# Feed-forward of a routed transformer block: w_out two pieces behind w_in, and two more banks for the first w_in pieces of a group

## What is computed

```python
# attention: q, k, v (4, 12, 448, 64)
attn = sigmoid(q @ k.T / 8 - log(448));  x = attn @ v        # -> (1792, 768)
# experts: each takes 224 tokens, the best logits first
logits = x @ w_gate                                          # (1792, 8)
for idx in argsort(-logits.flatten()):
    tok, e = idx // 8, idx % 8
    if assigned[tok] < 0 and counts[e] < 224: assigned[tok] = e; counts[e] += 1
for e in range(8):
    mask = assigned == e
    y[mask] = relu(x[mask] @ w1[e]) @ w2[e]                  # 768 -> 1024 -> 768
# feed-forward
h = y @ w_in                                                 # 768 -> 2048
g = max(h, 0) + alpha * min(h, 0)
out = g @ w_out                                              # 2048 -> 768
```

## Time and profile before

| | us |
|---|---|
| median of 3 runs (1068.49 to 1069.94) | 1068.9 |
| the profiled execution | 1074.37 |
| its span in the profile | 1072.7 |
| feed-forward of group 0, from its first product to its last | 133.5 |
| of group 1 | 124.7 |
| of group 2 | 124.5 |
| of group 3 | 118.3 |

### The profile page before, as it was taken

How to read it: one execution, slowest core, us unless ns; L and a number is a source line. 1 busy time by engine, 2 the same in 40 slices (tenths; PEclk the granted TensorE clock), 3 DMA queues, 4 the chain that set the end, 5 groups by cost and what they waited for, 6 DMA issues and landing times.

```text
span 1072.7 us, 16546 instructions
## 1 busy us (share of the span) xinstructions
PE 978.1 (91%) x6340; PEld 841.6 (78%) x6340; DVE 588.4 (55%) x1454; ACT 393.0 (37%) x628; POOL 185.5 (17%) x202
## 2 busy tenths in 40 slices
PE   5999999806969999799999999999999999999994
PEld 3555555406969898699989998998899999989993
DVE  2344444597765836966954586497539637211110
ACT  4676777401042123346312224542222355122212
POOL 0010110105150010233301014350100325100001
PEclk9999999956979999999999999999999999999997
DMA  9799997317379586847777855679685446966501
GB/s 213 204 260 270 275 264 228 135 35 236 103 206 363 191 221 181 285 128 223 265 280 235 239 177 130 190 222 368 208 241 195 151 129 188 375 231 220 177 1 51
DMA packets 121476, 222.32 MB, mean 207 GB/s; under 512 B 51424, under 2 KB 69216, under 8 KB 121408
## 3 DMA queue, kind: packets, MB, share of 16 engines
q1 hardware_dynamic: 88064, 120.34, 35.7%
q0 software_dynamic: 21280, 91.59, 27.4%
q10 hardware_dynamic: 12064, 9.47, 3.4%
HBM read 184.84 MB, written 36.52 MB: 206 GB/s over the span
## 4 chain that ended last, share of the span: by engine, by line
PE 83%; DVE 10%; ACT 2%; DMA 1%; issue 1%; POOL 0%; SPq 0%; ACTq 0%; DVEq 0%; POOLq 0%
PE psum L886 19%; PE psum L874 19%; PE psum L821 11%; PE psum L851 11%; PE psum L633 7%; PE psum L617 7%; DVE hits L1348 4%; PE psum L816 2%; PE psum L601 2%; PE psum L846 2%; PE psum L644 1%; DVE unit L1243 1%; DMA stage<-x_rows,tok_idx 1%; PE psum L768 1%; PE psum L652 1%
## 5 line engine op out<-in xcount | busy, mean ns | idle before, releaser
L886 PE MATMUL psum<-g_high,unit 128*128 128x448 f32 x768 | 231.7, 369 | 6.4 <-DVE g_low L1271 6.2
L874 PE MATMUL psum<-y_high,unit 128*128 128x448 f32 x768 | 231.5, 369 | 4.6 <-ACT below L1021 4.3
L886 PEld LDWEIGHTS psum<-g_high,unit 128*128 128x128 f32 x768 | 144.3, 188 | 21.8 <-DVE g_low L1271 9.9
L874 PEld LDWEIGHTS psum<-y_high,unit 128*128 128x128 f32 x768 | 144.3, 188 | 18.8 <-ACT below L1021 5.8
L874 PE MATMUL psum<-y_low,unit 128*128 128x448 f32 x384 | 140.5, 366 | 0.0
L886 PE MATMUL psum<-g_low,unit 128*128 128x448 f32 x384 | 140.5, 366 | 0.0
L1243 DVE TENSOR_TENSOR unit<-raw,unit 128x768 fp32r<-128x768 f32 (+1 forms) x106 | 109.3, 1060 | 39.7 <-ACT unit L994 39.2
L1020 ACT ACTIVATE above<-psum 128x448 f32<-128x448 f32 x64 | 35.0, 546 | 246.2 <-PE psum L874 246.2
L821 PE MATMUL psum<-x_high,unit 128*128 128x224 f32 x672 | 119.8, 280 | 2.9 <-DVE unit L1243 2.9
L1266 DVE SCALAR_TENSOR_TENSOR below<-below,neg_alpha,above 128x448 f32<-128x448 f32 x64 | 43.8, 684 | 138.1 <-ACT below L1021 137.7
L851 PE MATMUL psum<-h_high,unit 128*128 128x224 f32 x672 | 117.2, 278 | 2.5 <-issue 2.5
(11 more groups left out here) (159 smaller groups left out, 1278.7 us busy)
## 6 DMA issues: line engine op xcount, KB each, us to landing
unit<-ffn_parts SPq DMA_DIRECT2D x120, 768.0 KB, 6.4
ffn_parts<-pre_parts POOLq DMA_DIRECT2D x24, 768.0 KB, 5.7
ffn_parts<-unit SPq DMA_DIRECT2D x8, 768.0 KB, 5.5
q_in<-in_q_dram SPq DMA_DIRECT2D x24, 224.0 KB, 3.9
k_in<-in_k_dram SPq DMA_DIRECT2D x24, 224.0 KB, 5.9
v_in<-in_v_dram SPq DMA_DIRECT2D x24, 224.0 KB, 6.2
x_rows<-x_tok POOLq DMA_DIRECT2D x8, 672.0 KB, 5.5
rank_in<-suit_flat POOLq DMA_DIRECT2D x6, 896.0 KB, 14.2
```

Of the source, the lines that this page charges most:

```text
L874: last = pe.matmul(psum[:, IN_BANK, 0:PAIR], w, y[:, c, :], start=(c == 0 and i == 0), stop=(c == DC - 1 and i == 2))
L886: last = pe.matmul(psum[:, OUT_BANK + d, 0:PAIR], w, g[:, m % 2, :], start=(m == 0 and i == 0), stop=(m == FC - 1 and i == 2))
```

## The change

PE's order in a group becomes in 0, in 1, in 2, out 0, in 3, out 1, and so on to in 15, out 13, out 14, out 15. Piece 1 of w_in goes to bank 6 and piece 2 to bank 5, which belong to the result of w_out. So PE waits for `in_taken` only from piece 3 on (which waits that piece 2 is read), and ahead of the last two of the six result banks in out 0. On ACT, `take_in` of piece m now waits that g of piece m - 2 is split, and `round_g` of piece m waits that out m - 2 is done, since with the new order neither follows from what PE has done.

```diff
         def in_unit(q, m):
-            return STEPS * q + 2 * OWN + max(2 * m - 1, 0)
+            return STEPS * q + 2 * OWN + max(2 * m - 2, m)
         def out_unit(q, m):
-            return STEPS * q + 2 * OWN + min(2 * m + 2, 2 * FC - 1)
+            return STEPS * q + 2 * OWN + min(2 * m + 3, FC + m)
+        def in_bank(m):
+            return (IN_BANK, OUT_BANK + DC - 1, OUT_BANK + DC - 2)[m] if m < 3 else IN_BANK
...
             def ffn_in(q, m):
-                if m > 0:
+                if m > 2:
                     pe.wait_ge(in_taken, FC * q + m)
...
             def ffn_out(q, m):
                 for d in range(DC):
+                    if m == 0 and d == DC - 2:
+                        pe.wait_ge(in_taken, FC * q + 3)
...
                 for m in range(FC):
                     ffn_in(q, m)
-                    if m > 0:
-                        ffn_out(q, m - 1)
+                    if m > 1:
+                        ffn_out(q, m - 2)
+                ffn_out(q, FC - 2)
                 ffn_out(q, FC - 1)
...
             def take_in(q, m):
                 act.wait_ge(unit_used, in_unit(q, m) + 1)
+                if m > 1:
+                    act.wait_ge(g_split, FC * q + m - 1)
...
             def round_g(q, m):
                 act.wait_ge(g_made, FC * q + m + 1)
+                if m > 1:
+                    act.wait_ge(unit_used, out_unit(q, m - 2) + 1)
```

More of the change, by code:

```diff
@@ L363, in in_unit @@
         def in_unit(q, m):
-            return STEPS * q + 2 * OWN + max(2 * m - 1, 0)
+            return STEPS * q + 2 * OWN + max(2 * m - 2, m)
         def out_unit(q, m):
-            return STEPS * q + 2 * OWN + min(2 * m + 2, 2 * FC - 1)
+            return STEPS * q + 2 * OWN + min(2 * m + 3, FC + m)
+        def in_bank(m):
+            return (IN_BANK, OUT_BANK + DC - 1, OUT_BANK + DC - 2)[m] if m < 3 else IN_BANK
         def ffn_piece(u):
             k = u % STEPS - 2 * OWN
-            return 0 if k == 0 else 2 * FC - 1 if k == 2 * FC - 1 else 2 * ((k + 1) // 2) if k % 2 == 1 else k - 1
+            if k < 2:
+                return 2 * k
+            if k >= 2 * FC - 2:
+                return 2 * (k - FC) + 1
+            return k + 2 if k % 2 == 0 else k - 2
         def width(u):
@@ L873, in ffn_in @@
                     for i, (w, y) in enumerate(((w_high, y_high), (w_high, y_low), (w_low, y_high))):
-                        last = pe.matmul(psum[:, IN_BANK, 0:PAIR], w, y[:, c, :],
+                        last = pe.matmul(psum[:, in_bank(m), 0:PAIR], w, y[:, c, :],
                                          start=(c == 0 and i == 0), stop=(c == DC - 1 and i == 2))
@@ L1019, in take_in @@
                 act.wait_ge(unit_used, in_unit(q, m) + 1)
-                act.activation(above[:, m % 2, :], psum[:, IN_BANK, 0:PAIR], ACT.Relu)
-                act.activation(below[:, m % 2, :], psum[:, IN_BANK, 0:PAIR], ACT.Relu, scale=-1.0).then_inc(in_taken, 1)
+                if m > 1:
+                    act.wait_ge(g_split, FC * q + m - 1)
+                act.activation(above[:, m % 2, :], psum[:, in_bank(m), 0:PAIR], ACT.Relu)
+                act.activation(below[:, m % 2, :], psum[:, in_bank(m), 0:PAIR], ACT.Relu, scale=-1.0).then_inc(in_taken, 1)
             def round_g(q, m):
                 act.wait_ge(g_made, FC * q + m + 1)
+                if m > 1:
+                    act.wait_ge(unit_used, out_unit(q, m - 2) + 1)
                 act.copy(g_high[:, m % 2, :], below[:, m % 2, :]).then_inc(g_rounded, 1)
```

## The result

The changed kernel takes **1076.1 us** (median of 20 executions, 1070.7 to 1082.0) against 1071.1 (20 executions, 1068.2 to 1073.8) for the kernel before on the same chip: a ratio of **1.0055, 95% interval 1.0041 to 1.007**. It is slower, clear of noise: the medians are 5.0 us apart, and the ratio stands for 5.9 (4.4 to 7.5). The forecast was 0.27% faster, and slower had a chance of 0.05.

The account below looks back on a forecast made before the run. PE, 83% of the span, was taken as the bound through its waits and routing work. Group 3 -1.3, groups 1 and 2 0 each, group 0 -2.5, clock +0.9 make -2.9: 1066.0 us, range 1063.8 to 1068.2.

Parts of the forecast that it names:

- Group 3, -1.3: Feed-forward without routing: the 1.05 us wait before in 1 and one slow start of 0.26 go, gaining 1.3 us.
- Groups 1 and 2, 0 each: Per group, 2.9 us of waits and slow starts saved, 2.9 spent on new waits for flags; bounds -0.6 and +0.6.
- The new waits: PE waits for the flags in groups 1 and 2, since DVE's fill is late: 1.8 us, then 0.7.
- The 0.2 for what a wait costs beyond itself: At each new flags wait, some 0.2 us more, since the two small products run alone after a wait.
- waits of 1.7 never moved it: Argument that the clock stays full in group 0, giving 1065.1 us (1064.3 to 1065.9); chance 0.25.
- Group 0, -2.5: First feed-forward, its end set by DVE: 1.9 us earlier flags plus out 15's 0.4 + 0.26; bounds 0 and 3.4.
- The first pass for expert 3: DVE's pass in group 0 starts 1.1 us earlier on top of the threshold's 0.8, together 1.9.
- The wait at the second threshold: In group 0, PE arrives at 444.7 and thr_rows at 448.3: idle about 3.7 us, up to 4.4.
- The clock in group 0, +0.9: Half clock after PE's wait at the second threshold, partly covered by the flags wait, costs 0.9 us; bounds 0 and 2.9.
- I cost SP's and POOL's queues at nothing: Loads on both queues keep their rule and sizes and only trade places pairwise, so no cost was entered.
- The cover of eleven units: A piece is asked for eleven units ahead, some 40 us at 3.65 each, so loads should not make PE wait.
- The rival "slower": Group 0's PE stays at half clock some 20 us from the second threshold: +4.1, 1073 us; chance 0.05.

Follow-up runs that it names:

- e4: The changed kernel with DVE's weight splits of unit STEPS + 4 held until x has been gathered: 1071.2 us, ratio 0.9996 to the kernel before.
- e8: Changed kernel, w2 gathers first in group 0, fill one unit earlier in groups 1 and 2, idle filler products before group 0's threshold products: 1063.3 us, 0.9928.
- e3: The changed kernel with POOL's w2 gathers issued ahead of storing and spreading the logits, in group 0 only: 1068.9 us, ratio 0.9975.
- e0: The changed kernel once more, unedited, for a second profile: 1076.0 us, ratio 1.0048 to the kernel before.
- e9: e3 with fill one unit earlier in groups 1 and 2, plus e4's hold of DVE: 1060.6 us, ratio 0.9898 to the kernel before.

## Why the prediction was wrong

**Group 3, -1.3: right.** Measured -1.3 in the stretch, -1.4 to the end.

**Groups 1 and 2, 0 each: right in the sum and in the waits, and one cost missing.** The new waits were forecast at 1.8 and 0.7 and came at 1.68 and 0.70, then 1.75 and 0.71; ACT's order was read rightly. The 0.2 for what a wait costs beyond itself is what e4 shows. The pieces of 3.72 us, which the prediction counted as waits and routing work, stand on both sides alike. What was left out is the clock. The row of full clock through waits of 1.7 in the earlier trace rows was taken as a rule ("waits of 1.7 never moved it"). Four of ten such waits at the flags did move it, 1.7 us each: 1.4 us for an execution on average. The kernel before itself has such a fall, from 531.9 on for 3.4 us, behind a wait of 1.73 at L851, outside the stretches that I had looked at.

**Group 0, -2.5: right, measured -2.8.** The first pass for expert 3 starts 69.8 us into the stage in place of 71.8, 2.0 earlier, where 1.9 was forecast. The wait at the second threshold was 3.64, forecast 3.7, and the clock fell:

```profile
445.00:449.00 4.00, 4.00 (x14) 3.55 (x14) 3.80 (x11) 0.57 (x1) 0.00 (x0) 0.57 0.81 298
```

**The clock in group 0, +0.9: wrong place, and right in size by luck.** The fall at the second threshold costs about 0.2 (e8). But the first threshold's wait grew too, from 1.27 to 2.80. That follows from the prediction's own numbers (PE 2.1 earlier, `thr_rows` 0.8) and it was not followed up. In four of the eight profiled executions with the new order in group 0 and no filler, that wait took the clock down: 131.9 to 133.4 us for the stage, 130.3 to 130.7 in the others. On average that is about 1.0.

**"I cost SP's and POOL's queues at nothing": this is the step that failed.** The cover of eleven units was worked out for the pieces of w_in and w_out, which SP loads; PE never waits for one of those. POOL's queue was in the sentence, but not in the working. Its w2 gathers at the end of group 0 aren't asked for by a free slot alone. They stand in the queue behind work that hangs on DVE's routing, and the first piece of it, the gather of x, was held up by splits that the new order had moved beside it. The gathers came 3.5 us later into the stage, PE waited 4.10 and 0.81 us, and the clock fell. The term left out measured +6.3.

The sum with what was measured: -1.4 (group 3), -1.9 (group 0, averaged over the falls at the first threshold), +1.4 (falls behind the flags), +6.3 (handover) = +4.4, and measured was +5.0 by the medians and +5.9 by the ratio, with an interval of 4.4 to 7.5. So the sum is at the lower edge, and 0.6 to 1.5 us may have another source. The rival "slower" had the right sign for a wrong reason: PE's half clock in group 0 never lasted 20 us. e3, in which the handover costs nothing, comes out at 0.9975 against the 0.9973 forecast. In part that is luck: its handover is 1.0 shorter than before (71.1 against 72.1), which makes up for most of the 1.4 of falls that the forecast lacked.

## What to carry to other kernels

When a stage is made shorter, follow not only its own waits but every queue that feeds the next stage, up to the instruction at its head: what that instruction waits for may not come earlier, or may even come later, and when the room behind it is used up the next stage waits. Where the change moves work on DVE, look at what POOL issues at that time, for an indirect DMA can be held back by DVE's two-input instructions. And a wait of PE has a price beyond its length: 0.2 us here, and in some executions 1.7 more for the clock. When a difference is larger than the waits removed, compare the length of a piece that has no wait in it before the rest is put down to the stop.

## What the runs showed of the hardware

- An indirect DMA's issue on POOL took 0.93 us with DVE idle, 1.05 beside one short DVE instruction (`suit`, before) and 3.87 when DVE ran `TENSOR_TENSOR` with both inputs in SBUF; in three kernels (changed, e3, e4) it ended 0.8 us behind the last of these on DVE. A plain DMA's issue took 0.64 with and without one.
- TensorE went to half clock for 3.4 us behind waits of only 1.67 to 1.75 us, in some executions and not in others, at the same place of the same program (group 2: a wait of 1.75 without in the first profile of the changed kernel, one of 1.67 with in e0).
- A fall can be free: at the second threshold of group 0 (wait of 3.64 us, then 3.4 us at half clock) removing it gave 0.2 us (0 to 0.5 against four executions), because PE would have waited for the flags instead.
- A piece of 18 products took 3.65 us in some stretches and 3.72 in others, both at full clock and without idle time, and the stretches differ between executions of one program (group 3 of e3: all 32 pieces slow, 2.3 us).
- Gathers of w2 took a median of 11.9 us to land behind a load of 896 KB on the same queue (before), and 4.3 and 4.1 ahead of it (e8, e9).
